# A second buffer pair for block 22's transposed u, swapped PSUM banks for the last block and the first tile, and a recut order at the seam of two phases

## What is computed

```python
h = x @ w_in                                   # 3072 x 1024
e = np.exp(h - h.max(-1)); sm = e / (e.sum(-1) + 1e-9)
solu = h * sm
ln = (solu - mean) / np.sqrt(var + 1e-6) * g_ln
x2 = ln @ w_out                                # 3072 x 512
```

```python
e_idx = argmax(x2 @ w_gate)
y = np.maximum(x2[mask] @ w1[e], 0) @ w2[e]    # for each expert e
out[mask] = gate_w * sigmoid(x2 @ w_output_gate)[e] * y
```

## Time and profile before

| | |
|---|---|
| median of three runs | 775.51 us (773.63 to 777.45) |
| the profiled execution | 771.23 us |
| its span, first to last instruction | 769.5 us |
| TensorE busy | 738.9 us, 96% of the span |
| VectorE, ScalarE, GpSimd busy | 444.2, 303.6, 186.0 us |
| granted TensorE clock, mean | 0.992 |
| instructions | 16591 |

### The profile page before, as it was taken

The page is one execution under the profiler, slowest core; times in us unless marked ns, Lnnn a source line. Parts: engine busy times, 40 slices in busy tenths (PEclk is TensorE's granted clock), DMA queues, the critical chain, the costliest instruction groups (busy, mean ns, idle before and its releaser), DMA issues.

```text
span 769.5 us, 16591 instructions
## 1 busy us (share of the span) xinstructions
PE 738.9 (96%) x5512; PEld 644.5 (84%) x5513; DVE 444.2 (58%) x752; ACT 303.6 (39%) x466; POOL 186.0 (24%) x350
## 2 busy tenths in 40 slices
PE   2899999999999999999989999999999999999995
PEld 2799899989898998999878788888888888888884
DVE  4567678877867676767846736323646454544321
ACT  3424434444443444344325435224534444453220
POOL 4102435443321112112220312122121212212121
PEclk9989999999999999999999999999999999999998
DMA  9702442343223212312016444310535261601000
GB/s 290 275 0 71 145 146 97 96 160 127 69 81 124 69 69 89 117 69 69 29 43 236 163 154 152 129 55 23 177 113 205 94 243 54 245 23 46 22 27 21
DMA packets 22922, 84.98 MB, mean 110 GB/s; under 512 B 4078, under 2 KB 4334, under 8 KB 20976
## 3 DMA queue, kind: packets, MB, share of 16 engines
q1 hardware_dynamic: 16944, 67.66, 25.1%
q0 software_dynamic: 5952, 16.98, 7.1%
HBM read 73.74 MB, written 14.09 MB: 114 GB/s over the span
## 4 chain that ended last, share of the span: by engine, by line
PE 93%; DMA 3%; issue 1%; DVE 1%; POOL 1%; SPq 0%; DVEq 0%; ACT 0%; POOLq 0%; ACTq 0%
PE banks L1095 76%; PE banks L1240 3%; PE banks L1126 3%; PE banks L1145 3%; PE banks L1116 3%; PE banks L1108 2%; DMA k_sb<-k_win 2%; PE banks L1217 2%; PE banks L1167 1%; DMA stage<-w_both 1%; POOL win_lo L485 1%; SPq L409 0%; DVE uT_lo L793 0%; DVE he L804 0%; DVEq L395 0%
## 5 line engine op out<-in xcount | busy, mean ns | idle before, releaser
L1095 PE MATMUL banks<-slots_hi_lo,rT_hi 128*128 128x512 f32 x464 | 148.4, 401 | 0.2 <-issue 0.2
L1095 PE MATMUL banks<-slots_hi_lo,xsT_hi 128*128 128x512 f32 x464 | 124.5, 390 | 0.3 <-DVE xsT_lo L957 0.3
L1095 PEld LDWEIGHTS banks<-slots_hi_lo,xsT_hi 128*128 128x128 f32 x464 | 86.8, 188 | 18.6 <-issue 0.7
L1095 PEld LDWEIGHTS banks<-slots_hi_lo,rT_hi 128*128 128x128 f32 x464 | 83.1, 189 | 15.1 <-issue 0.4
L1095 PE MATMUL banks<-slots_hi_lo,rT_lo 128*128 128x512 f32 x232 | 90.8, 391 | 0.0
L556 POOL DMA_INDIRECT out<-ys,rows_out x29 | 30.1, 1039 | 238.5 <-DVE ys L1063 238.5
L1095 PE MATMUL banks<-wout_hi,uT_hi 128*128 128x264 f32 x384 | 82.7, 296 | 2.0 <-DVE uT_lo L793 2.0
L1055 DVE TENSOR_TENSOR slots_hi_lo<-raw_w,slots_hi_lo 128x1024 fp32r<-128x1024 f32 x56 | 65.0, 1223 | 27.5 <-ACT slots_hi_lo L724 27.5
L676 ACT ACTIVATE r_sb<-banks 128x1024 f32<-128x1024 f32 x29 | 29.7, 1026 | 123.9 <-PE banks L1095 123.9
L1095 PE MATMUL banks<-wout_hi,uT_lo 128*128 128x264 f32 x384 | 78.0, 285 | 0.0
L1095 PE MATMUL banks<-wout_lo,uT_hi 128*128 128x264 f32 x384 | 77.9, 284 | 0.0
(11 more groups left out here) (166 smaller groups left out, 1212.2 us busy)
## 6 DMA issues: line engine op xcount, KB each, us to landing
raw_w<-experts SPq DMA_DIRECT2D x14, 2048.0 KB, 7.3
k_sb<-k_win SPq DMA_DIRECT2D x24, 384.0 KB, 3.6
v_sb<-v_win SPq DMA_DIRECT2D x24, 384.0 KB, 4.8
x_rows<-x SPq DMA_DIRECT2D x24, 264.0 KB, 2.1
q_sb<-q_t SPq DMA_DIRECT2D x24, 256.0 KB, 2.7
stage<-experts POOLq DMA_DIRECT2D x8, 512.0 KB, 5.4
stage<-w_both SPq DMA_DIRECT2D x4, 512.0 KB, 7.0
wout_t<-w_out_t SPq DMA_DIRECT2D x1, 2048.0 KB, 13.0
```

The source lines that it names most:

```text
L1095: ins = mm(o, lhs, rhs(part, k, n), start=(k == first and lhs is not None and part == 0 and parts == (0, 1)), stop=(k == final and parts = ...
```

## The change

There are six edits. (1) Two new buffers `uT2_hi` and `uT2_lo` hold block 22's split u; all other blocks keep `uT_hi` and `uT_lo`, and block 23's `high_u` waits for `y_s` at 22 instead of 23. (2) Block 23's y goes to banks 0 and 1, and tile 0's h to banks 4 and 5; the waits follow: `product_out(23)` waits for `he_s` at 24, `hidden` of tile 0 for `x2_s` at 23, of tile 1 for `x2_s` at 24. (3) On TensorE the last chunk of `product_out(21)` is taken out of step 22 and stands behind `product_in(23)`; `u_turn(23)` comes behind chunk 4 of `product_out(22)` instead of chunk 6; three chunks of `product_out(23)` go ahead of `xs_turn(0)`; `ranks_late` goes one chunk forward. (4) On ScalarE `high_u(23)` goes ahead of `square_u(23)`. (5) On VectorE `copy_logits(21)` and `h_max(23)` go ahead of the second `one_hot`, and `solu(23)` ahead of `first_rows` and `late_base`. (6) `gate_max` of tiles 0 and 1 moves behind `low_r(1)`, and their `gate_exp` behind `pieces(0, 1)`.

```diff
--- before.py
+++ after.py
@@ -212,6 +212,10 @@
         nbi = {n: rb.take("nbi_" + n, [P, NBLK], I32) for n in ("rank", "q", "r")}
         first_tok = rb.take("first_tok", [P, EARLY, FIRST, 2], BF16)
         tile_bf = rb.take("tile_bf", [P, NBLK], BF16)
+        rb.at += (slot0 - rb.at) % (4 * BANK)
+        uT2_hi = rb.take("uT2_hi", [P, DF], F32R)
+        uT2_lo = rb.take("uT2_lo", [P, DF], F32R)
+        assert rb.at <= w2_lo.at
         place_hot = w2_lo.take("place_hot", [P, NBLK, P], BF16)
         assert w2_lo.at <= free_early_end
         tile_hot = w2_lo.take("tile_hot", [P, NBLK, NTILE], BF16)
@@ -247,14 +251,27 @@
         turn_ps = bank(2, 2)
         attn_ps = bank(2)
         y_ps = bank(4)
-        y2_ps = [bank(n)[:, 0:YB] for n in (4, 5)]
-        y_both = bank(4, 2).rearrange("p (b n) -> p b n", n=BANK)[:, :, 0:YB]
         fold_ps = bank(5)[:, 0:KF * 2 * E]
...
+
+        def static(t, *numbers):
+            return isinstance(t.i, int) and t.i in numbers
+
+        def uT(b):
+
+            return (uT2_hi, uT2_lo) if static(b, NBLK - 2) else (uT_hi, uT_lo)
+
+        def y_banks(b):
+
+            return bank(0 if static(b, NBLK - 1) else 4, 2)
+
+        def h_banks(t):
+
+            return bank(4 if static(t, 0) else 0, 2)
 
         def out_ps(t):
 
@@ -629,8 +646,8 @@
             def high_u(b):
 
                 act.wait_ge(uT_ps_s, b.i + 1)
-                at_least(act, y_s, b.i)
-                nc.scalar.activation(uT_hi[:, :], turn_ps, ACT.Copy).then_inc(uhi_s, 1)
+                at_least(act, y_s, b.i + (-1 if static(b, NBLK - 1) else 0))
+                nc.scalar.activation(uT(b)[0][:, :], turn_ps, ACT.Copy).then_inc(uhi_s, 1)
 
             def scale_y(b):
 
@@ -638,7 +655,8 @@
                 act.wait_ge(rstd_s, b.i + 1)
                 at_least(act, store_s[b.par], b.half * 16)
                 at_least(act, logc_s, b.i - 1)
-                nc.scalar.activation(x2[b.par][:, :].rearrange("p (h n) -> p h n", h=2), y_both, ACT.Copy,
+                nc.scalar.activation(x2[b.par][:, :].rearrange("p (h n) -> p h n", h=2),
+                                     y_banks(b).rearrange("p (b n) -> p b n", n=BANK)[:, :, 0:YB], ACT.Copy,
                                      scale=rstd[:, b.par:b.par + 1]).then_inc(x2_s, 1)
 
             def high_fold():
@@ -673,7 +691,7 @@
             def relu(t):
                 act.wait_ge(hid_s, t.i + 1)
                 at_least(act, rt_ps_s, t.i)
-                nc.scalar.activation(r_sb[:, :], h_ps, ACT.Relu).then_inc(relu_s, 1)
+                nc.scalar.activation(r_sb[:, :], h_banks(t), ACT.Relu).then_inc(relu_s, 1)
 
             def high_r(t):
 
@@ -698,16 +716,14 @@
             last = At(0, NBLK - 1)
             high_u(last + -1)
             exp_h(last)
+            high_u(last)
             square_u(last)
-            high_u(last)
             scale_y(last + -1)
             xt(At(0, 0))
             relu(At(0, 0))
             xt(At(0, 1))
             scale_y(last)
             high_r(At(0, 0))
-            gate_exp(At(0, 0))
-            gate_exp(At(0, 1))
             relu(At(0, 1))
             act.wait_ge(hot_s, 1)
             nc.scalar.activation(tile_tok[:, :, 1, :], tile_hot[:, :, :], ACT.Copy,
@@ -726,6 +742,8 @@
                 by_slot(act, e_next, emit)
 
             pieces(0, 1)
+            gate_exp(At(0, 0))
+            gate_exp(At(0, 1))
             xt(At(0, 2))
             last = last_tile(act)
             gate_exp(At(0, 2))
@@ -790,7 +808,8 @@
 
             def low_u(b):
                 dve.wait_ge(uhi_s, b.i + 1)
-                nc.vector.tensor_tensor(uT_lo[:, :], turn_ps, uT_hi[:, :].bitcast(F32), ALU.subtract).then_inc(ulo_s, 1)
+                hi, lo = uT(b)
+                nc.vector.tensor_tensor(lo[:, :], turn_ps, hi[:, :].bitcast(F32), ALU.subtract).then_inc(ulo_s, 1)
 
             def h_max(b):
                 dve.wait_ge(h_s, b.i + 1)
@@ -980,12 +999,12 @@
             one_hot(0, EARLY // 2)
             first_tokens()
             low_u(last + -1)
-            one_hot(EARLY // 2, EARLY)
             copy_logits(last + -2)
             h_max(last)
+            one_hot(EARLY // 2, EARLY)
+            solu(last)
             first_rows()
             late_base()
-            solu(last)
             low_u(last)
             copy_logits(last + -1)
             xt(At(0, 0))
@@ -993,8 +1012,6 @@
             copy_logits(last)
             dve.wait_ge(logc_s, NBLK)
             choose(EARLY, NBLK)
-            gate_max(At(0, 0))
-            gate_max(At(0, 1))
             low_r(At(0, 0))
 
             dve.wait_ge(rt_pe, 3)
@@ -1028,6 +1045,8 @@
             V.tensor_tensor(row_tbl[:, FIRST:NTILE], t32["row"][:, FIRST:], row_ps[:, NTILE + FIRST:2 * NTILE],
                             ALU.add).then_inc(tbl_s, 1)
             low_r(At(0, 1))
+            gate_max(At(0, 0))
+            gate_max(At(0, 1))
 
             link(V.tensor_tensor(et[:, :, :], blocks_wide(ne["end"][:, :], NTILE), wide(iota[:, 0:NTILE], E), ALU.is_le))
             link(V.tensor_reduce(t32["row"][:, :], et[:, :, :], AX.X, ALU.add))
@@ -1151,8 +1170,13 @@
                     pe.wait_ge(fold_lo_s, 1)
                 if 0 in chunks:
                     pe.wait_ge(ulo_s, b.i + 1)
-                    at_least(pe, x2_s, b.i)
-                last = split_product(y2_ps, lambda k: uT_hi[:, k * P:(k + 1) * P], lambda k: uT_lo[:, k * P:(k + 1) * P],
+                    if static(b, NBLK - 1):
+                        pe.wait_ge(he_s, NBLK)
+                    else:
+                        at_least(pe, x2_s, b.i)
+                hi, lo = uT(b)
+                outs = [y_banks(b)[:, n * BANK:n * BANK + YB] for n in range(2)]
+                last = split_product(outs, lambda k: hi[:, k * P:(k + 1) * P], lambda k: lo[:, k * P:(k + 1) * P],
                                      lambda part, k, n: (wout_hi, wout_lo)[part][:, k * YW + n * YB:k * YW + (n + 1) * YB],
                                      chunks, 0, KF - 1)
                 if KF - 1 in chunks:
@@ -1181,7 +1205,7 @@
                     scores(a + 1)
                 else:
                     ranks(0, EARLY)
-                product_out(c, range(5, KF))
+                product_out(c, range(5, KF - 1 if static(s, NBLK - 2) else KF))
 
             def ranks(lo, hi):
 
@@ -1223,10 +1247,12 @@
                     pe.wait_ge(w_ready[0], e * (W1C // CH) + 1)
                     pe.wait_ge(xtlo_s, t.i + 1)
                     at_least(pe, relu_s, t.i)
-                    if isinstance(t.i, int) and t.i == 0:
-                        pe.wait_ge(he_s, NBLK)
+                    if static(t, 0):
+                        pe.wait_ge(x2_s, NBLK - 1)
+                    if static(t, 1):
+                        pe.wait_ge(x2_s, NBLK)
                 def emit(slot):
-                    last = split_product([bank(0), bank(1)], lambda k: xsT_hi[:, k * P:(k + 1) * P], lambda k: xsT_lo[:, k * P:(k + 1) * P],
+                    last = split_product([h_banks(t)[:, n * BANK:(n + 1) * BANK] for n in range(2)], lambda k: xsT_hi[:, k * P:(k + 1) * P], lambda k: xsT_lo[:, k * P:(k + 1) * P],
                                          lambda part, k, n: slot[:, part * EW + k * DF + n * BANK:part * EW + k * DF + (n + 1) * BANK],
                                          chunks, 0, KD - 1)
                     if KD - 1 in chunks:
@@ -1246,8 +1272,6 @@
                     pe.wait_ge(w_ready[1], e * (W1C // CH) + 1)
                     pe.wait_ge(rtlo_s, t.i + 1)
                     at_least(pe, ys_s[t.par], t.half)
-                    if isinstance(t.i, int) and t.i == 0:
-                        pe.wait_ge(x2_s, NBLK)
 
                 def emit(slot):
                     last = split_product([out_ps(t)], lambda k: rT_hi[t.par][:, k * P:(k + 1) * P],
@@ -1277,19 +1301,22 @@
             product_in(last_b, range(0, 1))
             u_turn(last_b + -1)
             product_in(last_b, range(1, KD))
+            product_out(last_b + -2, range(KF - 1, KF))
             product_out(last_b + -1, range(0, 3))
             first_product()
-            product_out(last_b + -1, range(3, 7))
+            product_out(last_b + -1, range(3, 5))
             u_turn(last_b)
-            product_out(last_b + -1, range(7, KF))
+            product_out(last_b + -1, range(5, KF))
+            product_out(last_b, range(0, 3))
             xs_turn(At(0, 0))
-            product_out(last_b, range(0, 5))
+            product_out(last_b, range(3, 5))
             hidden(At(0, 0), range(KD))
             xs_turn(At(0, 1))
             product_out(last_b, range(5, KF))
             r_turn(At(0, 0))
-            hidden(At(0, 1), range(0, 2))
+            hidden(At(0, 1), range(0, 1))
             ranks_late()
+            hidden(At(0, 1), range(1, 2))
             hidden(At(0, 1), range(2, KD))
             expert_out(At(0, 0), range(0, 4), e=0)
             r_turn(At(0, 1))
```

## The result

The changed kernel is slower: 779.77 us median against 773.77 us for the kernel before on the same chip, 20 runs each, ratio 1.0079 (95% interval 1.0061 to 1.0096), that is +6.1 us. The forecast was 780.7 us, between 777.0 and 784.0, and +5.2 us in the difference. The profiled execution took 780.99 us with a span of 779.3, a mean granted clock of 0.983 (0.992 before).

What follows compares the result with a forecast made beforehand. TensorE, busy 738.9 of 769.5 us, was taken as the bound, so only its waits count. Terms 1.35 + 0.2 + 3.6 = 5.15, taken as +5.2 us on the 775.51 us median, gave 780.7 us, range 777.0 to 784.0.

Steps and rivals of the forecast that it cites:

- Part 1: Before product_out(22): the moved chunk delays scale_y(21) and high_u(22) behind it, a new TensorE wait of 3.13 us.
- Part 2: Block 23's chain: the wait before product_out(23) falls to 0.29 us, but hidden(0) starts 1.35 us later.
- Part 3: Swapped banks: hidden(1) waits 0.16 us for scale_y(23), ranks_late 0.04 for the hot table; +0.2 us.
- Part 4: Tile 2's turn: its gather waits for the moved gate_exp(0), a TensorE wait of 3.68 us; +3.6 us taken.
- A: Tile 2's gather wait is covered, leaving +1.55 us, 777.1 us; chance 0.07.
- B: Near 385 us high_u(22) is not held up, winning about 2.4 us; with the gather +1.2, 776.7 us; chance 0.05.
- C: The transposed u's waits vanish and the gather's 4 us disappear in slack: -2.7 us, 772.8 us; chance 0.03.
- D: The clock falls behind one of the two long TensorE waits: +7.2 to +8.2 us, about 783.2 us; chance 0.13.

Runs made afterwards that it cites:

- c1: The changed kernel with chunk 7 of block 21's product_out put back into step 22; ratio 1.0038 to the kernel before, +2.9 us.
- d2: The kernel before with only chunk 7 of block 21's product_out moved behind product_in(23); ratio 1.0065 to the kernel before, +5.0 us.
- d3: The changed kernel with gates put back, scale_y(21) behind high_u(22), and high_u(22) waiting for y_s at 21 only; ratio 0.9998 to the kernel before.
- c4: The changed kernel with useless products filling both waits, ahead of product_out(22) and tile 2's turn; ratio 1.0054 to the kernel before, +4.2 us.
- d1: The kernel before with only gate_max and gate_exp of tiles 0 and 1 moved; ratio 1.0077 to the kernel before, +6.0 us.
- d5: The kernel before timed and profiled again with no edit; ratio 1.0002 to the kernel before, +0.2 us.
- f4: The kernel before with 7 useless products in its 2.00 us wait ahead of product_out(23); ratio 0.9994 to the kernel before, -0.5 us.
- c3: The changed kernel with both the chunk and the gates put back; ratio 0.9973 to the kernel before, -2.1 us.
- c2: The changed kernel with gate_max and gate_exp of tiles 0 and 1 put back; ratio 1.0019 to the kernel before, +1.5 us.
- f2: The changed kernel with chunk, gates and VectorE's order around block 23 all put back; ratio 1.0003 to the kernel before, +0.2 us.

## Why the prediction was right, point by point

**Part 1, the late y.** Right in place, order and size: forecast a wait of 3.13 us at 388.48, measured 2.97 at 388.49 (390.22 - 1.73). c1, d2 and d3 show the cause.

**Part 2, the chain behind it.** `product_out(23)` waits 0.25 (forecast 0.29). The table's one-hot was no wait in after, because the half clock made TensorE itself late; in c4, with the clock up, it is 0.36 (forecast 0.42). `hidden(0)` was to be +1.35 later; it is +2.14 in after (25.55 - 23.41) and +1.44 in c4 (403.64 - 378.79 = 24.85). So the term for the waits was right and 0.7 us of the clock came on top.

**Part 3, the banks.** `scale_y(23)` ends at 412.97, `hidden(1)` starts at 413.12, bound by it as forecast. Forecast +1.55 in all up to `hidden(1)`, measured +1.76 in c4.

**Part 4, the gather.** The wait was to be 3.68, it is 3.75 in after, 3.69 in c1 and 3.78 in d1. The trace of after has no landing for this gather, but TensorE's start behind it bounds it: 429.19 to 432.80, at most 3.6 us, 3.55 if the release takes the 0.06 of before. That is near the median I took, with the DMA engines idle when it was issued (share 0.00 from 426 to 430 us). The estimate of 2.6 us, worked out from the Trainium skill (DMA: Bandwidth & Descriptors, section "Anatomy of one DMA — SWDGE (gpsimd) path"), was too short here.

**The rivals.** A, B and C did not come. B's mechanism is real (d3), but the change does not use it. D, the clock, which I gave 0.13 as something on top, came in every profile that had a wait of 2.96 us or more of TensorE at the seam, save where the wait was filled. The mis-sized term is this one, put at nothing in the sum. By the profiled pair alone the forecast is short: 776.4 was forecast, 780.99 measured. Of the 4.6 us between, 1.73 lie ahead of the seam and 3.3 in it (8.46 instead of 5.15, most of it the clock: 0.7 ahead of `hidden(0)`, and 2.1 between the turns of tiles 2 and 3, 10.04 us where it was 7.92), and the rest of the run gives 0.4 back. The 1.73 us ahead of the seam arise in the opening, whose steps the change leaves as they are. TensorE waits there for a load of keys. In the profile of before:

```profile
31.77 0.89 PE L1108 MATMUL banks<-k_sb,q_sb 64*64 64x96 f32 x32 [1.79 <-DMA k_sb<-k_win]
```

In that of after:

```profile
32.10 1.28 PE L1127 MATMUL banks<-k_sb,q_sb 64*64 64x96 f32 x32 [3.00 <-DMA k_sb<-k_win]
```

Behind the 3.00 us the clock of after is at 0.50 until about 35.8 us (1.71 us of full clock missing), behind the 1.79 us of before it stays at 1.00, and the first `u_turn` starts at 48.70 instead of 46.70. In d5, the kernel before again, it starts at 48.08, so the opening differs between executions of one kernel.

So the profile of before was one of its luckier executions on two counts, 771.23 us where its median over 20 runs is 773.77: a short opening, and no dip behind its 2.00 us wait, which costs 1.5 us at the seam where it comes (d5). The profile of after, with 780.99, is 1.2 us above its median. This fits with the medians lying closer to the forecast, +6.1 against +5.2, than the profiles do. Part of the agreement is thus two omissions that work against each other: the clock behind the new waits, and the clock behind the old one. How much each is worth in the medians is not shown, since c4 (1.9 us, intervals overlapping) and f4 (0.5 us, within the noise) leave it open. The 780.7 us itself came out closer than the shift by luck: its base, the median of three runs, was 1.7 us above the median of twenty, and the shift was 0.8 too small (5.2 for the 6.0 between the medians).

**The parts do not add exactly.** d1 + d2 + c3 is 6.0 + 5.0 - 2.1 = 8.9 us against 6.1 for after; the seams add better, 4.94 + 4.21 - 1.11 = 8.04 against 8.46. The intervals of d1 and d2 are some 1.7 us to each side, so I leave open whether there is an interaction. Taken each way, the gates' move costs 4.6 (after less c2), 5.0 (c1 less c3) and 6.0 us (d1), the chunk's 3.2 (after less c1), 3.6 (c2 less c3) and 5.0 us (d2).

## What to carry to other kernels

Before moving the last piece of a product, list who waits for its semaphore and what is queued behind those waiters on an engine that runs strictly in order: a second buffer frees nothing if an unrelated step ahead of it waits for the moved piece. A tiny instruction that frees a buffer for a transfer is worth the transfer's lateness, not its own length; look for it among the waits of the issuing engine before moving it behind long work. And put a stretch of half clock behind a new TensorE wait of 3 us into the sum (it was 1.7 us of full clock here, once 3.4), then check whether the profile you compare with had one of its own, at the seam or far from it.

## What the runs showed of the hardware that was not expected

A wait of 2.00 us among dense products brought the clock to half in one profile (d5) and not in another of the same kernel, and not in d1's or d2's; f2's wait of 2.15 us brought it down as well. Behind the six waits of 2.96 to 3.78 us at the seam (in after, c1, c2, d1, d2) it fell each time, and in c4, where products filled those waits, it did not; in d1, c1, c2, d2, d5 and f2 the stretch was 3.4 us at half rate, and in after it was 3.4 behind the first wait and 6.8 behind the second; why the second was longer than c1's and d1's behind like waits is open. The Trainium skill (TensorE: Matmul & The Clock Gate, Part 1) says that activity releases the throttled state, and the trace agrees: the clock came back each time while TensorE was working at half rate. A gather of 128 rows of 2112 bytes held TensorE until 3.6 us after its issue (in after and in d1, 425.87 to 429.51) although the load of expert 1's weights was over by then; the DMA's share was 0.00 when it was issued. Beside the tail of that load, in before, the landing had taken 3.8 us, so the quiet was worth little.
